# First layer's tokens in three parts of 384 instead of four of 288, with the pairs of heads taken alternately from the two halves of the tokens

## The chip, the cores and the metric

The kernel runs on one core of one Trainium2 chip. What counts is the device time of one execution in microseconds. The kernel before took 1,122.79 us, the median of 3 runs from 1,122.03 to 1,123.74.

The engines have short names: PE (TensorE, the matmuls), ACT (ScalarE), DVE (VectorE), POOL (GpSimd) and SP (SyncE, which issues most DMAs). PE reads its operands from SBUF and writes to PSUM, whose banks hold 512 float32 columns.

## What is computed

Three stages run in one kernel. Attention comes first, over 2 batches x 8 heads x 576 tokens x 64, causal, and mixed with a memory term by a gate per head. Its output is laid out as 1,152 tokens x 512 for a dense layer with a softplus between two matrices (the first layer below). Then come 8 experts, each weighted per token by a matrix P.

```
a = softmax(scale * q @ k.T, causal);  local = a @ v
mem_out = (phi(q) @ M_prev) / (phi(q) . z_prev + 1e-6);  g = 1 / (1 + exp(-beta))    # beta: one number per head
x = g * mem_out + (1 - g) * local                # [2, 8, 576, 64] -> [1152, 512]

h = x @ moe_w_in                                 # [1152, 2048]
y = (max(h, 0) + log1p(exp(-|h|))) @ moe_w_out   # [1152, 512]

P = exp(y @ w_gate - max), 8 times scaled by rows and columns
out = sum over e of P[:, e] * (max(y @ w1[e], 0) @ w2[e])
```

## The kernel before, in words

**Precision.** Every large product is made of three: each float32 operand is split into a rounded high part and the rest (`..h` and `..l`), and `products` issues high x high, high x low and low x high. ACT writes the high part (`copy`, L715), DVE or POOL the low part (`less`, L1029; POOL L655 for part of the experts' weights).

**Attention.** `pairs` runs over 8 pairs of heads (one pair fills 128 partitions), with a schedule written out by hand for each engine. The result of pair p is kept transposed in `xh[:, p, :]` and `xl[:, p, :]`, 576 tokens each. Before, pairs 0 to 3 are batch 0 and pairs 4 to 7 batch 1. ACT starts with three DMAs: two that bring `beta` to all partitions (L706), one per batch, and one for z (L707). Its first op is `gate_t` (L792), which waits for beta; DVE makes `gate_all` and `keep_all` from it (L1124 to L1131) before it takes up its first part of Q, `ql` (L1036). All later ACT ops are queued behind `gate_t`.

**First layer.** The loop is: 2 halves g of the 2,048 hidden features; in each, C1 = 4 chunks c of N1 = 288 tokens; in each chunk 8 tiles s of 128 features. `hidden1` makes the tile h of 128 features x 288 tokens in a bank of `ps_h` (12 matmuls), ACT and DVE compute the softplus (`soft_exp_ln`, `soft_sum`) and split it into `hh`, `hl` (`soft_hi`, `soft_lo`, a ring of 4), and `output1` adds its product with `moe_w_out` to four banks of `ps_y` (12 matmuls). PE's order is `hidden1` of tile n + 2, then `output1` of tile n; that is a step. At the end of a chunk DVE drains the four banks into `acc` (`drain_y`), and the first `output1` of the next chunk waits for that.

**What runs beside it.** The experts' part needs the first 512 tokens of y split in 7 forms (`xah`, `xal`: three quarters as they are, four sums that POOL makes in `token_sums`) and the first weights split (`weights_hi`, `weights_lo`, on POOL `weight_sums` and `weight_sums_lo`). Before, the tokens are split in steps 1 to 7 of the last chunk but one of g = 1 (kind "tokens"), and the weights in steps 1 to 3 of the last (kind "last"). In the last chunk's steps 6 and 7 there are no more tiles to make, and PE does the first products of the experts there: P1, P6, P5 before output 6, P2 and P7 before output 7, then P3 and P4 (`hidden2`). P1 and P2, and P4 with weights w = 2, wait for `c1_lo` of DVE, the others (P6 first) for `c1_los`, which POOL gives after L655. That op waits for part 2 of `weights_hi` on ACT.

The lines where a weight split waits or is waited for:

```
act.wait_ge(c1_sum, 4 * fp + 4)                            # weights_hi, part 2 (L856)
copy(w1c_h[i][:, 3:7, :, :], ws[:, :, :, :]).then_inc(c1_hi, 1)
pool.wait_ge(c1_hi, 3 * fp + 3)                            # weight_sums_lo (L654), then .then_inc(c1_los, 1)
pe.wait_ge(c1_los, 2 * s + i + 1)                          # hidden2, w >= 3 (L1607)
```

Of the kernel before, what the change touches and what calls it, by code (L numbers as in the profile page):

```python
# [12 lines left out]

P = 128
LAG = 2
RING = 4
MASKED = -1.0e30


# [48 lines left out]
def build(nc, q, k, v, M_prev, z_prev, beta, moe_w_in, moe_w_out, moe2_w_gate, moe2_w1, moe2_w2, out):  # L68
    B, H, S, D = q.shape
    DM = H * D  # L70
    KT = DM // P
    T = B * S
# [8 lines left out]
    FT = 8  # L81
    FS = FT * P
    G1 = moe_w_in.shape[1] // FS
    C1 = 4
    N1 = T // C1
    NTT = T // P
    M1 = C1 * FT
# [2 lines left out]
    SK_AT = [(1, "P4"), (2, "P7"), (2, "P4"), (3, "P4"), (4, "P7"), (4, "P4"), (5, "P4"), (6, "P7")]  # L90
    assert len(SK_AT) == SK
    SCALE = D ** -0.5
    assert D == 64 and 2 * D == P and TAIL == 64 and NQ == 9 and N1 * 2 == S and moe2_w1.shape[2] == FS
    NS, NB8, G = 5, 8, 2

    KEYS = [P, 2 * P, 3 * P, 4 * P, S]
# [14 lines left out]
    with ExitStack() as top:  # L111
# [75 lines left out]


        h_work, o = at_("h_work", X1, [P, 4, N1])
        assert 4 * N1 <= 2 * NJ * P  # L190
        W20 = o
        w2h, o = at_("w2h", W20, [P, FT, DM], F32R)
        w2l, o = at_("w2l", o, [P, FT, DM], F32R)
# [77 lines left out]
        BANK = {"P1": bank_a, "P2": bank_a, "P6": bank_b, "P7": bank_b, "P4": bank_b, "P5": bank_c, "P3": bank_c}  # L271
        width = lambda u: NA if u < 2 else NB
        XORDER = [0, 1, 2, 3, 4, 6, 5]
        XDONE = {x: n + 1 for n, x in enumerate(XORDER)}

        QUARTER = {"11": 0, "22": 1, "12": 2, "21": 3}
# [144 lines left out]

        PART_DONE = [1, 1, 2, 2, 3, 4, 5, 6, 8]

        def steps_of(t):

            return slice(2 * t, min(2 * t + 2, 9))
# [2 lines left out]
        @block.sync  # L429
        def _(sp):  # L430
            def load_heads(dst, src, pair, done):
                both = src[bass.ds(2 * pair, 2), :, :]
                for h in range(2):
                    sp.dma_start(dst[:, 0:NT, h * D:(h + 1) * D],
                                 src[bass.ds(2 * pair + h, 1), 0:NT * P, :].rearrange("o (j p) d -> p (o j) d", p=P))                        .then_inc(done, 16)
                sp.dma_start(dst[0:TAIL, NT, :].rearrange("p (h d) -> p h d", h=2),
                             both[:, NT * P:S, :].rearrange("h p d -> p h d")).then_inc(done, 16)

            def load_pair(pair, first=False):

                if first:
                    load_heads(q_nat, q3, pair, ld_q)
                else:
                    sp.wait_ge(phi_z, pair)
                    sp.dma_start(z_nat[:, pair % 2, :], z3[:, pair * P:(pair + 1) * P].broadcast_to([P, P]))\
                        .then_inc(ld_z[pair % 2], 16)
                    sp.wait_ge(t_ready, 5 * pair + 3)
                load_heads(k_nat, k3, pair, ld_k)
                if not first:
                    sp.wait_ge(phi_exp, pair + 1)  # L450
                    sp.wait_ge(phi_relu, pair + 1)
                    load_heads(q_nat, q3, pair, ld_q)
                    sp.wait_ge(v_split, 4 * pair + 4)
                else:
                    sp.wait_ge(nat_zeroed, 1)
                load_heads(v_nat, v3, pair, ld_v)
                for h in range(2):
                    sp.dma_start(mem_nat[h * D:(h + 1) * D, h * D:(h + 1) * D],
                                 m3[bass.ds(2 * pair + h, 1), :, :].rearrange("o p d -> p (o d)")).then_inc(ld_m, 16)
                if pair:  # L460
                    sp.wait_ge(ld_w1, 16 * pair)
                cols = slice(pair * P, (pair + 1) * P)
                sp.dma_start(raw1[:, :, cols], w1_dram(moe_w_in[:, cols])).then_inc(ld_w1, 16)
                sp.dma_start(raw2[:, pair, :], moe_w_out[cols, :]).then_inc(ld_w2, 16)
# [238 lines left out]
        def _(act):  # L703
            b2 = beta.rearrange("(o n) -> o n", o=1)
            for b in range(B):
                act.dma_start(beta_all[:, b * H:(b + 1) * H], b2.broadcast_to([P, H])).then_inc(ld_beta, 16)  # L706
            act.dma_start(z_nat[:, 0, :], z3[:, 0:P].broadcast_to([P, P])).then_inc(ld_z[0], 16)  # L707
            act.preload_act_table_set("natural_log_exp_and_others")
            act.sem_inc(t_hi, 5)
# [181 lines left out]
            def chunk(g, c, kind="", first=False):  # L891
                for s in range(FT):
                    n = g * M1 + c * FT + s
                    head = (s + LAG) % FT
                    ends = kind == "last" and g == G1 - 1
                    if not (ends and s + 1 >= FT):
                        soft_hi(n + 1, s + 1)
                    if not (ends and s + LAG >= FT):
                        soft_exp_ln(n + LAG, s + LAG)
                    if first and head == s + LAG:  # L900
                        split_w2(0, head)
                    if kind == "last" and not ends:
                        for tile in range(0 if s == 0 else s + LAG, min(s + LAG + 1, FT)):
                            split_w1(g + 1, tile, n - s + tile + 1)
                        if s >= 1:
                            split_w2(g + 1, s - 1, n + RING)
                    if kind == "tokens" and s >= 1:
                        if s == 1:
                            act.wait_ge(y_drained, KT * (C1 + 2) + KT)
                        tokens_hi(XORDER[s - 1], 0, NA, xah, xas, xa_sum, xa_hi)  # L910
                    if ends and 1 <= s <= 3:
                        weights_hi(0, 0, s - 1)
                    if ends and s == 4:
                        weights2_hi(0, 0)

            chunk(0, 0, "", True)
# [1 line left out]
                chunk(0, c)  # L918
            chunk(0, C1 - 1, "last")
            split_w2(1, FT - 1, M1 + RING)  # L920
            with act.Fori(0, C1 - 2) as c:
                chunk(1, c)
            chunk(1, C1 - 2, "tokens")
            chunk(1, C1 - 1, "last")

            def scale_first(s, u, tiles):
# [31 lines left out]
            tokens_b(3)  # L958
            copy_logits(2)
            tokens_b(4)  # L960
            copy_logits(3)
            tokens_b(6)
            tokens_b(5)

# [47 lines left out]
        def _(dve):  # L1012
# [232 lines left out]
            def chunk(g, c, kind="", first=False):  # L1245
                for s in range(FT):
# [8 lines left out]
                    if kind == "last" and not ends:  # L1255
                        for tile in range(0 if s == 0 else s + LAG, min(s + LAG + 1, FT)):
                            split_w1(g + 1, tile)
                        if s >= 1:
                            split_w2(g + 1, s - 1)
                    if kind == "tokens" and s >= 1:  # L1260
                        tokens_lo(XORDER[s - 1], 0, NA, xah, xal, xas, xa_sum, xa_hi, xa_lo)
                    if ends and 1 <= s <= 2:
                        weights_lo(0, 0, s - 1)
                    if ends and s == 4:
                        weights2_lo(0, 0)
                if not ends:
                    drain_y(g, c)
# [3 lines left out]
                chunk(0, c)  # L1271
            chunk(0, C1 - 1, "last")
            split_w2(1, FT - 1)
            with dve.Fori(0, C1 - 2) as c:
                chunk(1, c)
            chunk(1, C1 - 2, "tokens")
            chunk(1, C1 - 1, "last")

            sum_u2(0, 0)
# [143 lines left out]
        def _(pe):  # L1423
# [127 lines left out]
            def hidden1(n, slot, c, tile, stage):  # L1551

                pe.wait_ge(h_read, n + 1)
                pe.wait_ge(w1_lo, FT * stage + tile + 1)
                for kt in range(KT):
                    at_ = bass.ds((c // 2) * (HPB * S) + kt * S + (c % 2) * N1, N1)
                    last = products(ps_h[:, slot % 2, 0:N1], (w1h[:, tile, kt, :], w1l[:, tile, kt, :]),
                                    [x[:, :, :].rearrange("p a b -> p (a b)")[:, at_] for x in (xh, xl)],
                                    kt == 0, kt == KT - 1)
                last.then_inc(h_ready, 1)  # L1560
# [205 lines left out]
```

## Time and profile before

| | |
|---|---|
| median of 3 runs | 1,122.79 us |
| profiled execution | 1,121.92 us |
| its span, first to last instruction | 1,120.1 us |
| mean granted clock of PE | 0.998 |
| PE busy | 1,106.3 us, 99% |
| DVE, ACT, POOL busy | 707.2, 502.2, 433.7 us |
| chain that ended last | PE 95%, DVE 2%, issue 1%, POOL 1% |

The span is 1.8 us shorter than the execution's own time; what lies around it isn't in the trace. The share of busy time says which engine is full, and the chain of waits says what each piece of work came after. Along the program there are four stretches: a start up to about 26 us, attention to 146 us, the first layer to 354 us, and the experts. One chunk of the first layer lasts about 25.4 us. A DMA row of the page gives the time from issue to landing, not the time that its packets take.

### The profile page before, as it was taken

To read this page: it belongs to the slowest core of one execution; us is meant where nothing else is said; L and a number is where in the kernel's file an instruction comes from. 1 tells how busy PE (TensorE), PEld (TensorE's weight loads), DVE (VectorE), ACT (ScalarE), POOL (GpSimd) and SP (SyncE) were. 2 spreads that over 40 slices of the span, in tenths; PEclk is the share of its full clock that TensorE was granted. 3 is DMA by queue.
4 is the path that set the end of the run, shared out by engine and by line. 5 is a ranking of instruction groups with operands and counts; after the bars stand their busy time and mean duration, and the time that the engine had idled before them with its cause. 6 is when DMAs were issued, how large, how long until landed. Compare 5 with 4: busy or idle time off the path is not lost.

```text
span 1120.1 us, 21542 instructions
## 1 busy us (share of the span) xinstructions
PE 1106.3 (99%) x7114; PEld 1006.7 (90%) x7114; DVE 707.2 (63%) x1359; ACT 502.2 (45%) x1126; POOL 433.7 (39%) x487
## 2 busy tenths in 40 slices
PE   6999999999999999999999999999999999999998
PEld 4888899999998988999998989989899899898997
DVE  6988743363357787666656667565675656657564
ACT  5888765585566333532333323333233333333331
POOL 6988700000116243353434434244252442524421
PEclk9999999999999999999999999999999999999999
DMA  4343112002001011101111011110111101111001
GB/s 110 92 103 100 38 70 75 1 1 77 0 0 57 20 57 39 57 20 57 57 37 56 19 56 56 37 56 19 56 56 37 50 25 56 50 38 43 19 10 76
DMA packets 65934, 52.79 MB, mean 47 GB/s; under 512 B 32480, under 2 KB 53984, under 8 KB 65888
## 3 DMA queue, kind: packets, MB, share of 16 engines
q1 hardware_dynamic: 65456, 52.13, 15.2%
q8 instruction: 25, 0.41, 0.2%
q14 instruction: 21, 0.17, 0.0%
q10 hardware_dynamic: 432, 0.07, 0.0%
HBM read 49.83 MB, written 2.36 MB: 47 GB/s over the span
## 4 chain that ended last, share of the span: by engine, by line
PE 95%; DVE 2%; issue 1%; POOL 1%; DMA 0%; ACT 0%; SPq 0%; ACTq 0%; POOLq 0%; DVEq 0%
PE ps_y L1464 40%; PE ps_h L1464 27%; PE ps_g L1464 17%; PE ps_o L1464 5%; PE ps_p L1502 2%; PE ps_s L1478 2%; PE ps_y L1696 1%; PE ps_s L1464 0%; DMA k_nat<-in_k_dram 0%; DVE zl L1226 0%; PE ps_t L1445 0%; DVE acc L1345 0%; PE ps_t L1456 0%; PE ps_t L1449 0%; POOL prob L594 0%
## 5 line engine op out<-in xcount | busy, mean ns | idle before, releaser
L889 ACT ACTIVATE zh<-h 128x256 fp32r<-128x256 f32 (+1 forms) x256 | 112.2, 444 | 328.7 <-POOL h L667 133.6
L1464 PE MATMUL ps_y<-w2c_h,zh 128*128 128x512 f32 x512 | 202.7, 396 | 0.0
L1464 PE MATMUL ps_y<-w2c_l,zh 128*128 128x512 f32 x512 | 201.8, 394 | 0.0
L1464 PE MATMUL ps_y<-w2c_h,zl 128*128 128x512 f32 x512 | 199.4, 389 | 0.0
L662 POOL TENSOR_TENSOR h<-u,p 128x256 f32<-128x256 f32 (+1 forms) x64 | 56.9, 889 | 350.6 <-DVE u L1203 350.6
L1226 DVE SCALAR_TENSOR_TENSOR zl<-h,zh 128x256 fp32r<-128x256 f32 (+1 forms) x256 | 173.0, 681 | 8.5 <-ACT zh L889 6.3
L1464 PEld LDWEIGHTS ps_y<-w2c_h,zl 128*128 128x128 f32 x512 | 96.2, 188 | 21.9
L1464 PEld LDWEIGHTS ps_y<-w2c_h,zh 128*128 128x128 f32 x512 | 96.6, 189 | 13.4
L1464 PEld LDWEIGHTS ps_y<-w2c_l,zh 128*128 128x128 f32 x512 | 96.6, 189 | 11.8
L1353 DVE SCALAR_TENSOR_TENSOR acc<-ps_y,weight,acc 128x512 f32<-128x512 f32 x112 | 82.1, 741 | 37.2 <-PE ps_y L1464 37.2
L667 POOL TENSOR_TENSOR h<-h,p 128x256 f32<-128x256 f32 (+1 forms) x64 | 61.0, 952 | 101.3 <-DVE h L1214 101.3
L655 POOL TENSOR_TENSOR w1c_l<-ws,w1c_h 128x1024 fp32r<-128x1024 f32 x32 | 76.8, 2401 | 27.9 <-ACT w1c_h L715 27.9
L1156 DVE SCALAR_TENSOR_TENSOR h_work<-ps_h,h_work 128x288 f32<-128x288 f32 x64 | 29.3, 457 | 88.5 <-ACT h_work L823 88.5
L1464 PE MATMUL ps_h<-xbh,w1c_l 128*128 128x320 f32 x256 | 79.1, 309 | 0.0
L1464 PE MATMUL ps_h<-xbl,w1c_h 128*128 128x320 f32 x256 | 79.0, 309 | 0.0
L1464 PE MATMUL ps_h<-xbh,w1c_h 128*128 128x320 f32 x256 | 78.7, 307 | 0.0
L1464 PE MATMUL ps_h<-xh,w1h 128*128 (+1 forms) x256 | 75.6, 295 | 0.0
L1464 PE MATMUL ps_y<-hh,w2h 128*128 128x288 f32 x256 | 75.5, 295 | 0.0
L1464 PE MATMUL ps_y<-hh,w2l 128*128 128x288 f32 x256 | 75.5, 295 | 0.0
L1464 PE MATMUL ps_h<-xh,w1l 128*128 (+1 forms) x256 | 75.5, 295 | 0.0
L1464 PE MATMUL ps_y<-hl,w2h 128*128 128x288 f32 x256 | 75.4, 294 | 0.0
L1464 PE MATMUL ps_h<-xl,w1h 128*128 (+1 forms) x256 | 75.4, 294 | 0.0
(243 smaller groups left out, 3049.6 us busy)
## 6 DMA issues: line engine op xcount, KB each, us to landing
rc<-in_moe_w_dram SPq DMA_DIRECT2D x64, 512.0 KB, 3.6
out_dram<-acc SPq DMA_DIRECT2D x9, 256.0 KB, 2.0
q_nat<-in_q_dram SPq DMA_DIRECT2D x16, 128.0 KB, 2.5
k_nat<-in_k_dram SPq DMA_DIRECT2D x16, 128.0 KB, 2.9
v_nat<-in_v_dram SPq DMA_DIRECT2D x16, 128.0 KB, 2.4
raw<-in_moe_w_in_dram SPq DMA_DIRECT2D x8, 256.0 KB, 3.0
raw<-in_moe_w_out_dram SPq DMA_DIRECT2D x8, 256.0 KB, 3.1
raw<-in_moe_w_in_dram SPq DMA_DIRECT2D x1, 2048.0 KB, 7.8
```

The costliest lines, as they stand in the source:

```text
L655: pool.tensor_tensor(w1c_l[i][:, 3:7, :, :], ws[:, :, :, :], w1c_h[i][:, 3:7, :, :].bitcast(F32), ALU.subtract).then_inc(c1_los, 1)
L662: pool.tensor_tensor(h22[:, 0:n], u3[:, 0:n], p5[:, 0:n], ALU.add).then_inc(h22_done, 1)
L667: pool.tensor_tensor(h12[:, 0:n], h12[:, 0:n], p5[:, 0:n], ALU.add).then_inc(h12_done, 1)
L889: act.activation(z_place(u, quarter, 0), rows, ACT.Relu).then_inc(e_hi, 1)
L1156: dve.scalar_tensor_tensor(out=h_sp[:, slot % 2, :], in0=ps_h[:, slot % 2, 0:N1], scalar=0.0, in1=h_abs[:, slot % 2, :], op0=ALU.max, op1= ...
L1226: dve.scalar_tensor_tensor(out=z_place(u, quarter, 1), in0=rows[:, 0:n], scalar=0.0, in1=z_place(u, quarter, 0).bitcast(F32), op0=ALU.max, ...
L1353: dve.scalar_tensor_tensor(out=here, in0=y, scalar=weight[:, i, bass.ds(e, 1)], in1=here, op0=ALU.mult, op1=ALU.add).then_inc(z_drained, 1)
L1464: last = pe.matmul(dst, a[x], b[y], start=start and i == 0, stop=stop and i == 2)
L1478: pe.matmul(ps_s[:, bank + h, 0:w], x[r, half, t * P:(t + 1) * P], y[r, half, 0:w], start=i == 0, stop=False)
L1502: last = pe.transpose(ps_p[:, b % 2, at_:at_ + P], rows, ident[:, :])
L1696: last = pe.matmul(bank[0:E, 0:N1], wg[:, kt, :], y1[:, kt, c * N1:(c + 1) * N1], start=kt == 0, stop=kt == KT - 1)
```

## The change

C1 goes from 4 to 3 and N1 from 288 to 384, so the first layer has 48 tiles instead of 64. A chunk of 384 no longer ends where a batch ends (576), so the tokens of both batches must lie one behind the other: pairs are taken as batch 0, batch 1, batch 0, batch 1 (`place_of`), and the pair's number gives its place in `xh`, `xl`. The gates are used by the pair's number, so `beta_all` is filled in that order too: one DMA per batch still, now with a third dimension on both sides. The ring of `hh`, `hl` has 2 places. `h_work` grows from 4,608 to 6,144 bytes per partition. The tokens are split in the last chunk itself, up to two forms in a step (`TOKENS_AT`), and the weights two steps later than before.

```diff
-RING = 4
+RING = 2
-    C1 = 4
+    C1 = 3
-        assert 4 * N1 <= 2 * NJ * P
+        assert 4 * N1 <= 3 * NJ * P
+        TOKENS_AT = [0, 0, 2, 4, 6, 7, 7, 7, 7]
+        def place_of(pair):
+            return pair % B * (NP // B) + pair // B
             def load_heads(dst, src, pair, done):
+                pair = place_of(pair)
...
             for b in range(B):
-                act.dma_start(beta_all[:, b * H:(b + 1) * H], b2.broadcast_to([P, H])).then_inc(ld_beta, 16)
+                act.dma_start(beta_all[:, :].rearrange("p (k b h) -> p k b h", b=B, h=2)[:, :, b, :],
+                              b2.rearrange("o (k h) -> o k h", h=2).broadcast_to([P, HPB, 2])).then_inc(ld_beta, 16)
...
-                    if kind == "tokens" and s >= 1:
-                        if s == 1:
-                            act.wait_ge(y_drained, KT * (C1 + 2) + KT)
-                        tokens_hi(XORDER[s - 1], 0, NA, xah, xas, xa_sum, xa_hi)
-                    if ends and 1 <= s <= 3:
-                        weights_hi(0, 0, s - 1)
-                    if ends and s == 4:
+                    if ends and s == 1:
+                        act.wait_ge(y_drained, KT * (C1 + 2) + KT)
+                    if ends:
+                        for x in XORDER[TOKENS_AT[s]:TOKENS_AT[s + 1]]:
+                            tokens_hi(x, 0, NA, xah, xas, xa_sum, xa_hi)
+                    if ends and 3 <= s <= 5:
+                        weights_hi(0, 0, s - 3)
+                    if ends and s == 6:
                         weights2_hi(0, 0)
...
-                    at_ = bass.ds((c // 2) * (HPB * S) + kt * S + (c % 2) * N1, N1)
+                    at_ = bass.ds(kt * T + c * N1, N1)
```

The same edits stand in DVE's chunk (`tokens_lo`, `weights_lo`, `weights2_lo`); one `copy_logits` goes.

ACT's queue at the end of the first layer, before: from the second part of the first weights to their second matrix (`w1c_h_110<-ws` is part 2 of `weights_hi`; `hh<-h_work` is `soft_hi`, and the three ops on `h_work` are `soft_exp_ln`).

```order
L715 ACTIVATE w1c_h_110<-rc_0_127 128x256
L715 ACTIVATE hh<-h_work 128x288
L819 ACTIVATE h_work<-ps_h 128x288
L821 ACTIVATE h_work<-h_work 128x288
L823 ACTIVATE h_work<-h_work 128x288
L715 ACTIVATE w1c_h_110<-ws 128x1024
L715 ACTIVATE hh<-h_work 128x288
L819 ACTIVATE h_work<-ps_h 128x288
L821 ACTIVATE h_work<-h_work 128x288
L823 ACTIVATE h_work<-h_work 128x288
L715 ACTIVATE w2c_h_132<-rc_0_129 128x1024
L715 ACTIVATE hh<-h_work 128x288
```

The same stretch now:

```order
L723 ACTIVATE w1c_h_110<-rc_0_127 128x256
L723 ACTIVATE hh<-h_work 128x384
L827 ACTIVATE h_work<-ps_h 128x384
L829 ACTIVATE h_work<-h_work 128x384
L831 ACTIVATE h_work<-h_work 128x384
L723 ACTIVATE w1c_h_110<-ws 128x1024
L723 ACTIVATE hh<-h_work 128x384
L723 ACTIVATE w2c_h_132<-rc_0_129 128x1024
L723 ACTIVATE s_119<-ps_h 128x256
L723 ACTIVATE w1c_h_115<-rc_1_128 128x512
L723 ACTIVATE w1c_h_115<-rc_1_128 128x256
L723 ACTIVATE p_120<-ps_h 128x256
```

Before, three `hh` and six ops on `h_work` stood between part 2 and `s_119<-ps_h` (what ACT takes from P1), beside the second matrix; now one `hh` and the second matrix are left between them. Part 2 follows the softplus of the last tile instead of that of the last but two.

ACT's first rows, before:

```order
L706 DMA beta_all<-in_beta_dram 128x8 x2
L707 DMA z_nat<-in_z_prev_dram 128x128
L708 ACT_TABLE_LOAD
L792 ACTIVATE gate_t<-beta_all 128x16
L715 ACTIVATE qh<-ps_t 128x512
```

and now:

```order
L713 DMA beta_all<-in_beta_dram 128x4x2 x2
L715 DMA z_nat<-in_z_prev_dram 128x128
L716 ACT_TABLE_LOAD
L800 ACTIVATE gate_t<-beta_all 128x16
L723 ACTIVATE qh<-ps_t 128x512
```

Nothing moves there; the shape of beta's two loads goes from 128x8 to 128x4x2, and `gate_t` still stands ahead of everything else on ACT.

## Rows read from the trace of the kernel before

**Rows 1.** The page: busy time of PE over the span, its share and matmuls

```profile
PE 1106.3 (99%) x7114; PEld 1006.7 (90%) x7114; DVE 707.2 (63%) x1359; ACT 502.2 (45%) x1126; POOL 433.7 (39%) x487
```

**Rows 2.** Busy time by stage: stretch, us, busy us of each engine, PEclk, DMA

```profile
8.20:11.50 3.30, 3.26 (x12) 2.41 (x12) 1.65 (x4) 2.09 (x7) 0.00 (x0) 0.50 0.62 191
...
26.00:146.25 120.25, 118.91 (x1015) 104.83 (x1014) 100.55 (x239) 97.29 (x274) 98.87 (x153) 1.00 0.37 97
146.25:353.97 207.72, 207.72 (x1567) 207.12 (x1568) 98.57 (x202) 131.94 (x296) 16.66 (x15) 1.00 0.09 29
...
449.30:1117.00 667.70, 667.60 (x3894) 601.83 (x3893) 415.48 (x718) 225.12 (x453) 262.10 (x246) 1.00 0.13 43
```

**Rows 3.** Chain of work in the first layer: start us, us, engine, tile, line, matmuls

```profile
254.89 1.60 PE ps_y L1464 x12
256.49 1.58 PE ps_h L1464 x12
...
328.03 1.78 PE ps_y L1464 x12
```

**Rows 4.** Chain of work later: matmuls of 256, 320 and 512 columns

```profile
345.77 0.72 PE ps_h L1464 x6
346.49 0.72 PE ps_g L1464 x6
...
374.92 0.88 PE ps_g L1464 x6
...
446.55 2.75 PE ps_y L1464 x12
```

**Rows 5.** PE in time, attention stage: pairs of 384 columns, half the rows each

```profile
64.86 0.35 PE L1478 MATMUL ps_s<-kl,qh 64*128 64x384 f32 x2
65.04 0.35 PE L1478 MATMUL ps_s<-kh,ql 64*128 64x384 f32 x2
```

**Rows 6.** ACT in time, last chunk, the step that holds w1c_h<-ws

```profile
337.83 0.41 ACT L819 ACTIVATE h_work<-ps_h 128x288 f32<-128x288 f32 x1 [0.85 <-PE ps_h L1464]
...
339.10 1.04 ACT L715 ACTIVATE w1c_h<-ws 128x1024 fp32r<-128x1024 f32 x1
```

**Rows 7.** POOL in time, from the tokens' sums to the weights' low part

```profile
302.86 1.44 POOL L632 TENSOR_TENSOR xas<-acc 128x512 f32<-128x512 f32 x1 [165.15 <-DVE acc L1243]
...
311.24 1.06 POOL L651 TENSOR_TENSOR ws<-rc,ws 128x256 f32<-128x256 f32 x1
340.22 2.40 POOL L655 TENSOR_TENSOR w1c_l<-ws,w1c_h 128x1024 fp32r<-128x1024 f32 x1 [27.93 <-ACT w1c_h L715]
```

**Rows 8.** All engines in time at the start

```profile
5.29 0.21 ACT L792 ACTIVATE gate_t<-beta_all 128x16 f32<-128x16 f32 x1 [1.84 <-DMA beta_all<-in_beta_dram]
...
6.67 0.18 DVE L1131 TENSOR_SCALAR keep_all<-gate_all 128x16 f32<-128x16 f32 x1
...
8.24 0.69 DVE L1036 SCALAR_TENSOR_TENSOR ql<-ps_t,qh 128x512 fp32r<-128x512 f32 x1 [1.40 <-ACT qh L715]
8.24 1.11 PE L1449 MATMUL ps_o<-ident,k_nat 128*128 128x128 f32 x4 [0.72 <-DMA k_nat<-in_k_dram]
...
10.02 0.69 DVE L1029 TENSOR_TENSOR kl<-ps_o,kh 128x512 fp32r<-128x512 f32 x1 [1.09 <-ACT kh L715]
...
11.42 0.42 PE L1478 MATMUL ps_s<-kh,qh 64*128 64x256 f32 x2
```

**Rows 9.** DMA queues in 1.75 to 5.20 us: packets, MB, share

```profile
q1 hardware_dynamic: 1089, 0.27, 34.9%
q10 hardware_dynamic: 366, 0.05, 7.3%
```

**Rows 10.** DMA issues up to 20 us: count, KB each, median us to landing

```profile
q_nat<-in_q_dram SPq DMA_DIRECT2D x4, 128.0 KB, 2.8
...
z_nat<-in_z_prev_dram SPq DMA_DIRECT2D x1, 64.0 KB, 3.4
beta_all<-in_beta_dram ACTq DMA_DIRECT2D x2, 4.0 KB, 3.4
```

More of the change, by code:

```diff
@@ L92, in build @@
     SCALE = D ** -0.5
-    assert D == 64 and 2 * D == P and TAIL == 64 and NQ == 9 and N1 * 2 == S and moe2_w1.shape[2] == FS
+    assert D == 64 and 2 * D == P and TAIL == 64 and NQ == 9 and N1 * C1 == T and B == 2 and moe2_w1.shape[2] == FS
     NS, NB8, G = 5, 8, 2
@@ L444, in load_pair @@
                     sp.wait_ge(phi_z, pair)
-                    sp.dma_start(z_nat[:, pair % 2, :], z3[:, pair * P:(pair + 1) * P].broadcast_to([P, P]))\
+                    sp.dma_start(z_nat[:, pair % 2, :], z3[:, place_of(pair) * P:(place_of(pair) + 1) * P].broadcast_to([P, P]))\
                         .then_inc(ld_z[pair % 2], 16)
@@ L458, in load_pair @@
                     sp.dma_start(mem_nat[h * D:(h + 1) * D, h * D:(h + 1) * D],
-                                 m3[bass.ds(2 * pair + h, 1), :, :].rearrange("o p d -> p (o d)")).then_inc(ld_m, 16)
+                                 m3[bass.ds(2 * place_of(pair) + h, 1), :, :].rearrange("o p d -> p (o d)")).then_inc(ld_m, 16)
                 if pair:
@@ L920, in _ @@
             split_w2(1, FT - 1, M1 + RING)
-            with act.Fori(0, C1 - 2) as c:
+            with act.Fori(0, C1 - 1) as c:
                 chunk(1, c)
-            chunk(1, C1 - 2, "tokens")
             chunk(1, C1 - 1, "last")
@@ L960, in _ @@
             tokens_b(4)
-            copy_logits(3)
             tokens_b(6)
@@ L1259, in chunk @@
                             split_w2(g + 1, s - 1)
[L1260 to L1264, printed above, removed]
+                    if ends:
+                        for x in XORDER[TOKENS_AT[s]:TOKENS_AT[s + 1]]:
+                            tokens_lo(x, 0, NA, xah, xal, xas, xa_sum, xa_hi, xa_lo)
+                    if ends and 3 <= s <= 4:
+                        weights_lo(0, 0, s - 3)
+                    if ends and s == 6:
                         weights2_lo(0, 0)
@@ L1273, in _ @@
             split_w2(1, FT - 1)
-            with dve.Fori(0, C1 - 2) as c:
+            with dve.Fori(0, C1 - 1) as c:
                 chunk(1, c)
-            chunk(1, C1 - 2, "tokens")
             chunk(1, C1 - 1, "last")
```

## Prediction

> **What bounds the kernel now.** I read the page first: PE is busy 99% of the span [rows 1]. Busy time by stage then says where that is loose [rows 2]. The attention stage after 26 us leaves PE 1.3 us idle in 120, the first MoE layer (146 to 354 us) leaves nothing at a granted clock of 1.00, and the expert loop from 449 us leaves 0.1 in 668. Only the start is loose: from 8.2 to 11.5 us the clock is 0.50, the 1.2 GHz level, and PE there runs fillers while it waits. So a change pays if it takes PE time out of a dense stage, and costs if it puts a wait into one. A late start costs in full as well, since no dense stage can catch up. The third view, the chain of waits, shows pieces of 12 matmuls with nothing between them in the first layer; two of its pieces are late, by 0.15 and 0.19 us [the second is in rows 3], both where a chunk begins and DVE still drains the last one.
>
> **Part 1: 384 columns for 288.** Every tile of the first layer takes 12 matmuls to make (`ps_h`) and 12 to use (`ps_y`). Before, there are 2 x 4 x 8 = 64 tiles, 1,536 matmuls; now 2 x 3 x 8 = 48, 1,152. The columns streamed are the same, 442,368. A piece of 12 at 288 columns takes 1.58 to 1.60 us [rows 3], 132.5 ns each. At the 2.4 GHz of clock 1.00 the columns are 120 ns of that; 12.5 ns are per matmul. The sum before is 1,536 x 132.5 = 203.5 us.
> No row has a full matmul of 384 columns. From below: the same 12.5 ns on top of 160 gives 172.5 ns, 198.7 us, a gain of 4.8. From above: two matmuls of 384 columns on half the rows each follow one another in 0.18 us [rows 5]; 178 ns gives 205.1 us, a loss of 1.6. The nearest rows are the full ones: 320 columns at 0.88/6 = 146.7 ns and 512 at 2.75/12 = 229.2 ns [rows 4]. 384 lies a third of the way: 174.1 ns, 200.6 us. I take this: **-2.9 us**.
> On what a matmul costs beyond its columns the Trainium skill disagrees: "TensorE: Matmul & The Clock Gate", section "Back-to-back issue gap", puts the gap of isolated matmuls at the columns over 2.4 GHz plus about 2.5 ns. By that, 384 fewer matmuls would be worth 1.0 us; the pieces of [rows 3] show five times that overhead where each matmul has its own weights, and the measurement decides.
> The two late pieces of 0.34 us together should go: a step (two pieces) is 4.2 us instead of 3.2, while DVE's work in it grows by a fixed-cost share only, and the chunk before the last has no token splits any more. **-0.3 us**, bounds 0 and -0.4.
> The smaller ring for `hh`/`hl` (2 for 4) costs nothing: the tile n+1 is split after tile n-1 is used, and between lie three pieces of PE work, 6.3 us, against some 1.1 us for the two splits. The waits on `h_read` already hold ACT to that pace. The gate's logits have the same columns in 3 groups as in 4; their fewer instructions are under 0.1 us. Fewer y drains (24 for 32) are hidden either way. The order of pairs changes addresses only, and the first layer's first chunk needs pairs 0, 2, 4 and 6, all done when `hidden1` starts.
>
> **Part 2: the tail of the first layer.** The token splits (14 ops of 512 elements on ACT and DVE) now share the last chunk with the weight splits, and these move from its steps 1 to 3 to steps 3 to 5. What waits for them: PE's product P6, in step 6, needs `c1_los`, which POOL gives after `w1c_h<-ws` on ACT. Before, POOL was done at 340.22 + 2.40 = 342.62 and P6 started at 346.49 [rows 4, 7]: 3.9 us in hand. Two steps later there is none. From the time that the step's `hidden1` ends: ACT starts 0.04 us later, reaches the weights 1.27 us after that [rows 6], plus 3 x 0.08 for three wider ops (96 elements; 0.41 us at 288), copies 1.04, POOL starts 0.08 later and takes 2.40. Together 5.1 us. PE has until then one output piece, 12 x 174 = 2.1 us, and P1, 0.72 [rows 4]: 2.8 us. So P6 waits **+2.3 us**. Bounds: 0 if the weights came otherwise early (I see no way), 3.2 if ACT runs behind. ACT's fullest step (3) has 4 ops of about 0.5, two tokens and one weight split of 0.6, 3.9 us of 4.2; step 4 and 5 are light, so it catches up. POOL's sums for the tokens and weights take 302.86 to 312.3 [rows 7], 9.4 us, and are needed first in step 2, one sum, and last in step 5, 21 us into the chunk: covered. Behind `c1_los` on POOL stand the sums for the second weights, 4.2 us, needed only after P3 and P4 and under the logits. What DVE does in that time (`hl` of tile 7, the weights' low part) has PE's pieces P6, P5 and output 6 as cover.
>
> **Part 3: the start.** ACT's two beta loads were 128 runs of 8 numbers; to interleave the two batches each is now 128 x 4 runs of 2 numbers. The bytes are the same, 4 KB each [rows 10]; the packets go from 256 of 32 B to 1,024 of 8 B. ACT waits for them before its first op: at 5.29 us [rows 8], and this wait was the DMA's. Then DVE makes the gates until 6.85, and only then `ql`, at 8.24. The path that sets the start is not this one but `k_nat`, which lands at 8.2 [rows 8].
> How late may beta be? If ACT starts at T, gates are made at T + 1.6, `ql` and `kl` take 0.69 each, the two `qtl` and the last `kl` 0.7 together, and the first scores (11.42 now) start at about T + 3.7. So the start slips by T - 7.7, and by nothing below.
> T isn't in the trace. From 1.75 to 5.20 us the ACT queue moved 366 packets, 106 per us, beta's among them, beside 1,089 of SP's [rows 9]. Bounds: by bytes, T stays 5.3 and the slip is 0. By count times the whole time to landing (3.45 us x 4 + 1.75 = 15.6), the slip is 7.9. At the queue's rate, 1,024 packets need 9.7 us, T is 11.8 with 0.3 for the last signal, the slip 4.0. In favour of counting packets: a z load of 128 packets, all from one row of DRAM as beta's are, takes 3.4 us to land, while a q load of 512 packets and twice the bytes takes 2.8 [rows 10]. I take the middle one: **+4.0 us**. It is also the largest term and the least certain. PE's fillers end at 11.4, so its clock may fall again to the 1.2 GHz level before the scores; up to 1 us more, not in the sum.
>
> **Sum.** -2.9 - 0.3 + 2.3 + 4.0 = +3.1 us on the profiled execution's 1,121.92 us (its span is 1,120.1): 1,125.0. The median of the runs, 1,122.79, is 0.9 above that execution; carried over, 1,125.9.
>
> **Rivals.**
> A. Beta lands early enough (T below 7.7). For it: both loads are 8 KB together, and in the same stretch SP's queue moved three times as many packets as ACT's [rows 9], so the DMA engines can do more than ACT's queue asked of them. Against it: the rates of [rows 9]. Then -0.9: 1,121.9, no change; with the 384 columns at their lower bound, 1,120.0, faster.
> The Trainium skill speaks for this one: "DMA: Bandwidth & Descriptors", section "Why small descriptors are slow (HBM only)", charges about 3 cycles of a bus per packet and 32 bytes of descriptor, by which 48 more packets on each of 16 engines would be an estimated fraction of a us, and the start would not move. No row here shows packets of 8 bytes.
> B. Packets decide in full and hold up SP's loads too: slip 7.9, +7.0 in all, 1,129.8. For it: SP's queue ran at 316 packets per us beside beta. Against: it lets the fixed part of the time to landing grow with the count, too.
> C. P6 finds its weights ready, and beta is early: -3.2, 1,119.6. Against it stands the order of ACT's work; it needs two errors.
> D. 384 columns cost 178 ns: +4.5 on the forecast, 1,130.4. Only pairs that share the array show it.
>
> **How the numbers follow.** Forecast 0.45, A 0.30, B 0.15, C 0.05, D 0.05. A difference under 0.2%, 2.2 us, can't be told from none: faster is below 1,120.5, slower above 1,125.0. The forecast's case spreads with T, 1,123.5 to 1,128: slower 0.8, same 0.2. A: same 0.75, faster 0.25. B and D slower, C faster. So faster 0.08 + 0.05 = 0.13; same 0.09 + 0.22 = 0.31; slower 0.36 + 0.15 + 0.05 = 0.56. The range takes in most of A and B: 1,119.8 to 1,130.5; the forecast's own is 1,123.5 to 1,128.
>
> **What would show it.** Pieces of 12 at 384 columns take 2.07 to 2.09 us. ACT's `gate_t` starts at about 11.8 us with its wait put down to beta's DMA, and the first scores at 15.5. PE has one wait in the last chunk, before P6, 2.3 us, released by POOL. The expert loop is unchanged. The forecast is wrong if `gate_t` starts before 7.7 us, or if P6 starts right behind P1.

## The result and the profile after

| | before | after |
|---|---|---|
| median | 1,122.79 us (5 runs, 1,122.03 to 1,123.77) | 1,129.84 us (5 runs, 1,127.79 to 1,131.12) |
| span of the profiled execution | 1,120.1 us | 1,127.7 us |
| ratio, after to before | | 1.0061, 95% interval 1.0050 to 1.0073 |

The changed kernel is slower, by 7.05 us in the medians and 7.6 us in the spans of the two profiled executions. PE does a little less work than before and waits more; this is the page, with PE's busy time and the granted clock in 40 slices, to be read beside [rows 1]:

```profile
PE 1105.4 (98%) x6722; PEld 1005.4 (89%) x6722; DVE 700.6 (62%) x1319; ACT 489.3 (43%) x1061; POOL 434.9 (39%) x487
...
PEclk9999999999999999999999999999999999999999
```

The clock reads 9 in all 40 slices of 28 us; what is shorter has to be looked for in smaller stretches. PE's busy time fell by only 0.9 us, which already says that something ate what the wider tiles gave. By stage (stretch, us, then busy us and instructions of PE, PEld, DVE, ACT and POOL, PEclk, DMA share, GB/s), beside [rows 2]:

```profile
8.20:14.60 6.40, 0.00 (x0) 0.02 (x1) 0.42 (x2) 0.22 (x1) 0.00 (x0) 1.00 0.40 84
...
34.00:154.80 120.80, 119.77 (x1020) 105.85 (x1018) 100.63 (x238) 97.97 (x274) 98.85 (x153) 1.00 0.36 95
154.80:361.61 206.81, 204.53 (x1184) 204.19 (x1184) 91.89 (x162) 119.06 (x232) 17.36 (x15) 0.99 0.09 29
```

From 8.2 to 14.6 us PE now does nothing (the 1.00 of its clock there is no reading, see the end). Attention and the first layer are as dense as before, but for 2.3 us in the second.

The chain of waits (start us, us, engine, tile, matmuls), beside [rows 3, 4]:

```profile
161.25 2.08 PE ps_h L1471 x12
...
349.05 2.36 POOL w1c_l L662
351.45 1.65 PE ps_g L1471 x6
354.38 2.29 PE ps_y L1471 x12
```

A piece of 12 matmuls at 384 columns takes 2.08 us, 173.3 ns each, where 288 took 1.59 us. Then the last chunk's P6 (`ps_g`) comes behind a POOL op, and its six matmuls take 1.65 us instead of 0.72; the next output piece takes 2.29 instead of 2.08. PE's longest waits (engine, line, what it waited for, total us, times, longest):

```profile
PE ps_t L1452 <- DMA q_nat<-in_q_dram: 10.2, 1, 10.2
PE ps_g L1471 <- POOL w1c_l L662: 2.3, 1, 2.3
```

And the start, engines in order of time, beside [rows 8]: SP's issue of v, ACT's `gate_t`, PE's first transposes of q, the first scores:

```profile
6.71 4.97 SPq L441 DMA_DIRECT2D v_nat<-in_v_dram  x2
...
13.78 0.22 ACT L800 ACTIVATE gate_t<-beta_all 128x16 f32<-128x16 f32 x1 [10.05 <-DMA beta_all<-in_beta_dram]
...
14.61 1.09 PE L1452 MATMUL ps_t<-ident,q_nat 128*128 128x128 f32 x4 [10.17 <-DMA q_nat<-in_q_dram]
...
18.94 0.58 PE L1485 MATMUL ps_s<-kh,qh 64*128 64x256 f32 x2
```

`gate_t` is 8.5 us late, q itself lands 7.7 us later than before, and the scores start 7.5 us later. The DMA queues in the first stretch of [rows 9] (packets, MB, share of 16 engines' time), and then from 8.2 to 11.5 us:

```profile
q1 hardware_dynamic: 528, 0.13, 16.6%
q10 hardware_dynamic: 331, 0.00, 4.3%
```

```profile
q10 hardware_dynamic: 348, 0.01, 5.4%
q1 hardware_dynamic: 77, 0.02, 2.4%
```

ACT's queue moves about 96 packets per us in the first stretch and 105 in the second, of 8 bytes, as it moved 106 of mostly 32 bytes before. SP's queue fell from 1,089 packets to 528 in the first stretch, and from 1,039 to 77 in the second, with its share of the engines' time at 2.4%: the queue is not busy, it is held up. SP's own issue of v took 4.97 us for two DMAs, against 1.48 us in the kernel before; that its queue did not drain is the likely reason.

Put together from the profiled executions. The first deep attention piece on `ps_o` moved from 40.69 to 48.72 us: +8.0. 1,152 x 173.3 ns against 1,536 x 132.5 is -3.9, two late drains -0.3. P6 started 2.4 us after P1's last matmul would have let it, and behind it the slow clock cost 1.5 (6 matmuls of P6 and 6 of P5 took 2.73 us, start to start, instead of 1.43, at about 0.21 us each but the first, and the output piece lost 0.25 us). The sum is +7.7 us; the spans differ by 7.6.

### The profile page after: what moved, and what is told of

Read it like the earlier page. It is cut to its first block, busy times and chain, and to the rows that moved or that the text cites. A ratio compares the mean times of both kernels' runs of the same rounds, so it can differ in the third digit from the quotient of the medians.

```text
span 1127.7 us, 20453 instructions
## 1 busy us (share of the span) xinstructions
PE 1105.4 (98%) x6722; PEld 1005.4 (89%) x6722; DVE 700.6 (62%) x1319; ACT 489.3 (43%) x1061; POOL 434.9 (39%) x487
## 4 chain that ended last, share of the span: by engine, by line
PE 93%; DVE 2%; issue 1%; DMA 1%; POOL 1%; ACT 1%; SPq 0%; ACTq 0%; POOLq 0%; DVEq 0%
PE ps_y L1471 39%; PE ps_h L1471 26%; PE ps_g L1471 17%; PE ps_o L1471 4%; PE ps_p L1509 2%; PE ps_s L1485 2%; DMA k_nat<-in_k_dram 1%; PE ps_s L1471 0%; PE ps_y L1703 0%; DVE zl L1233 0%; PE ps_t L1452 0%; PE ps_t L1456 0%; DVE acc L1352 0%; PE ps_g L1703 0%; PE ps_t L1463 0%
## 5 line engine op out<-in xcount | busy, mean ns | idle before, releaser
L1471 PEld LDWEIGHTS ps_y<-w2c_l,zh 128*128 128x128 f32 x512 | 96.6, 189 | 11.8
L1163 DVE SCALAR_TENSOR_TENSOR h_work<-ps_h,h_work 128x384 f32<-128x384 f32 x48 | 26.8, 558 | 99.3 <-ACT h_work L831 99.2
L1471 PE MATMUL ps_h<-xah,w1c_l 128*128 128x256 f32 x256 | 72.7, 284 | 0.0
L1471 PE MATMUL ps_h<-xal,w1c_h 128*128 128x256 f32 x256 | 72.6, 284 | 0.0
L1471 PE MATMUL ps_h<-xah,w1c_h 128*128 128x256 f32 x256 | 72.4, 283 | 0.0
L1227 DVE TENSOR_TENSOR h<-ps_g,u 128x256 f32<-128x256 f32 (+1 forms) x64 | 29.3, 458 | 64.5 <-PE ps_g L1471 64.3
L723 ACT ACTIVATE s<-ps_h 128x256 f32<-128x256 f32 (+1 forms) x64 | 26.3, 410 | 97.0 <-PE ps_h L1471 96.9
```

The source lines that it names most:

```text
L723: copy = lambda o, i, **kw: act.activation(o, i, ACT.Copy, **kw)
L1163: dve.scalar_tensor_tensor(out=h_sp[:, slot % 2, :], in0=ps_h[:, slot % 2, 0:N1], scalar=0.0, in1=h_abs[:, slot % 2, :], op0=ALU.max, op1= ...
L1227: dve.tensor_tensor(h21[:, 0:n], bank_b[:, 0:n], u3[:, 0:n], ALU.add).then_inc(h21_done, 1)
L1471: last = pe.matmul(dst, a[x], b[y], start=start and i == 0, stop=stop and i == 2)
```

## The experiments

Two theories had to be told apart from their rivals. One: beta's packets alone made the start late, not the new order of the pairs. Two: the wait for P6 costs more than its own length, since the clock falls behind it. Four runs took the changed kernel apart, four put beta's loads into the kernel before, three followed what these showed. Each is compared with the kernel before on the same chip (medians 1,122.7 to 1,123.0). The edits are cut to the lines that matter; the semaphore counts at their ends are left out.

### Beta in 32-byte runs again, all else changed

```diff
-                act.dma_start(beta_all[:, :].rearrange("p (k b h) -> p k b h", b=B, h=2)[:, :, b, :],
-                              b2.rearrange("o (k h) -> o k h", h=2).broadcast_to([P, HPB, 2]))
+                act.dma_start(beta_all[:, b * H:(b + 1) * H], b2.broadcast_to([P, H]))
...
-            act.activation(gate_t[:, :], beta_all[:, :], ACT.Exp, scale=-1.0)
+            act.activation(gate_t[:, :].rearrange("p (k b h) -> p k b h", b=B, h=2),
+                           beta_all[:, :].rearrange("p (b k h) -> p k b h", b=B, h=2), ACT.Exp, scale=-1.0)
```

> The changed kernel, but beta comes as before (two loads of 128 runs of 32 bytes, 256 packets) and gate_t's access pattern puts the numbers in the new order. Theory S (beta's 1,024 small packets made the start late): gate_t starts at 5.3 us as before, the first scores at 11.4 instead of 18.9, and the time falls by the 8.0 us that the start slipped, to 1,121.9. Rival (the start is late by the new order of the pairs, whose loads come from other places in DRAM): q, k still land late, 1,129.8. The tail of the first layer stays as it is: P6 waits 2.3 us.

Measured: 1,122.75 us (11 runs), ratio to the kernel before 0.9992 (0.9983 to 1.0001). ACT's `gate_t` and the first scores:

```profile
5.49 0.21 ACT L799 ACTIVATE gate_t<-beta_all 128x16 f32<-128x16 f32 x1 [2.03 <-DMA beta_all<-in_beta_dram]
...
11.39 0.39 PE L1486 MATMUL ps_s<-kh,qh 64*128 64x256 f32 x2
```

The time is 0.9 us above what was expected, but the scores start where they did, with the pairs in the new order. So the start's slip was beta's packets, and the rest of the change together is worth nothing that can be told, as the terms -3.9, -0.3, +2.4 and +1.5 add up to -0.3. (In this profiled execution the first deep `ps_o` piece comes at 41.80 us, 1.1 later than in that of the kernel before, and at 41.28 in that of the run with both edits below. The granted clock goes with it: its mean from 11.5 to 34 us is 0.85 here, 0.92 in the run with both edits (whose records of the clock begin at 13.0 us) and 1.00 in the kernel before. So part of this is likely PE's clock in the loose stretches of the start; no run tells the order of the pairs apart from it.)

### Weights split one step earlier, beta still slow

```diff
-                    if ends and 3 <= s <= 5:
-                        weights_hi(0, 0, s - 3)
-                    if ends and s == 6:
+                    if ends and 2 <= s <= 4:
+                        weights_hi(0, 0, s - 2)
+                    if ends and s == 5:
                         weights2_hi(0, 0)
```

(and the same for `weights_lo` and `weights2_lo` on DVE)

> The changed kernel with the first weights split in steps 2 to 4 of the last chunk instead of 3 to 5 (the second matrix in step 5). Beta stays slow. POOL's low part then ends about 1.9 us before P6 is due. Theory W (the wait for it costs 2.3 us itself and about 1.5 more, since PE's clock drops to the 1.2 GHz level behind the wait and the next 18 matmuls run at it): P6 starts right behind P1 at full clock and the time falls by 3.9 us, to 1,125.9. Rival (only the wait counts, the slow matmuls come from something else in that place, such as POOL and DVE at the same memory): it falls by 2.3, to 1,127.5, with P6 still at 0.21 us per matmul of 256 columns.

Measured: 1,125.88 us (10 runs), ratio 1.0024 (1.0014 to 1.0033), 4.0 us below the changed kernel. P1 and P6 in the chain (`ps_h`, `ps_g`, six matmuls each):

```profile
348.55 0.71 PE ps_h L1471 x6
349.26 0.72 PE ps_g L1471 x6
```

P6 starts right behind P1 and both run at 0.12 us per matmul. Four us is the wait and its slow matmuls, not the wait's 2.4 alone. POOL (`ws<-rc`) and DVE (`hl`, `w2c_l`) have the same kind of work beside P6 as in the changed kernel, so the slow matmuls were not theirs.

### Both edits

> Both edits on the changed kernel: beta in 32-byte runs, the weights split one step earlier. What is left of the change against the kernel before is the 384 columns and the later chunk's ends: 1,152 matmuls at 173.3 ns are 199.7 us against 203.5, and two late drains of 0.34 go: 4.1 us below the kernel before, 1,118.7. If the gain of the wider tiles is lost elsewhere too (rival), it stays within 2 us of 1,122.8.

Measured: 1,118.63 us (5 runs), ratio 0.9961 (0.9947 to 0.9974): 4.4 us below the kernel before in the medians. P1 and P6 in the chain:

```profile
341.04 0.71 PE ps_h L1472 x6
341.75 0.72 PE ps_g L1472 x6
```

This is the change without its two costs, and the gain is what 384 fewer matmuls and two drains were reckoned at. Between this run and the first of the four stands only the place of the weight splits: 1,122.75 against 1,118.63, 4.1 us.

### Filler matmuls in the wait

The first experiment's kernel, and between P1 and P6:

```diff
-                        hidden2(0, 0, ("P1", "P6", "P5"))
+                        hidden2(0, 0, ("P1",))
+                        for _ in range(10):
+                            pe.matmul(bank_b[:, :].rearrange("p (k n) -> p k n", k=2), w1c_h[0][:, 0, 0, :],
+                                      xah[:, 0, :, :], start=True, stop=True)
+                        hidden2(0, 0, ("P6", "P5"))
```

> As the first of these four (beta in 32-byte runs, weights late), with ten matmuls of 512 columns between P1 and P6 that write to P6's bank and are thrown away: 2.2 us of PE work, where PE waited 2.3 us. Their results aren't used, so the output is the same. Theory W (the clock drops because PE is idle): P6 starts at the same time as without them but at full clock, and the time is 1.5 us below that kernel. Rival (the matmuls behind the wait are slow for another reason): P6 at 0.21 us per matmul as before, the same time.

Measured: 1,121.46 us (11 runs), ratio 0.9984 (0.9975 to 0.9993); 1.3 us below the kernel without fillers. The fillers' row (ten matmuls of 512 columns, merged), a matmul of P6 behind them, and one of the output piece:

```profile
341.64 2.45 PE L1690 MATMUL ps_g<-xah,w1c_h 128*128 128x512 f32 x10
...
344.37 0.28 PE L1472 MATMUL ps_g<-xal,w1c_h 128*128 128x256 f32 x1
...
345.86 0.34 PE L1472 MATMUL ps_y<-hl,w2h 128*128 128x384 f32 x1
```

The same stretch without fillers: the first matmul of P6, one of P5, one of the output piece and one after it:

```profile
344.55 0.39 PE L1472 MATMUL ps_g<-xah,w1c_h 128*128 128x256 f32 x1 [2.28 <-POOL w1c_l L662]
...
345.65 0.42 PE L1472 MATMUL ps_h<-xah,w1c_l 128*128 128x256 f32 x1
...
347.79 0.52 PE L1472 MATMUL ps_y<-hl,w2h 128*128 128x384 f32 x1
...
349.19 0.33 PE L1472 MATMUL ps_y<-hh,w2h 128*128 128x384 f32 x1
```

With fillers a matmul of 256 columns takes 0.28 us and one of 384 takes 0.34 (start to end; they overlap); without, 0.42 and 0.52, from about 1 us after P6's start until one of 384 is back at 0.33, at 349.19. The granted clock goes with it: 0.50 from 345.5 to 346.8 us without fillers, and 1.00 from 341.6 to 349.4 with them. The 10 useless matmuls save 1.3 us, so it is PE's idling before them, not what other engines do, that makes them slow.

### The kernel before with 8-byte runs of beta

```diff
-                act.dma_start(beta_all[:, b * H:(b + 1) * H], b2.broadcast_to([P, H]))
+                act.dma_start(beta_all[:, :].rearrange("p (k b h) -> p k b h", b=B, h=2)[:, :, b, :],
+                              b2.rearrange("o (k h) -> o k h", h=2).broadcast_to([P, HPB, 2]))
```

Beta's loads are those of the changed kernel, and `gate_t` puts the gates back into the old order.

> The kernel before with nothing changed but beta's loads: 1,024 packets of 8 bytes as in the changed kernel, put in order by gate_t's access pattern. Theory S: gate_t at 13.8 us, q landing at 14.6, first scores at 18.9, total 8.0 us over the kernel before, 1,130.8. Rival (the order of the pairs has a part in the late start): less than that.

Measured: 1,130.07 us (4 runs), ratio 1.0063 (1.0046 to 1.0080), 7.2 us over the kernel before.

```profile
13.66 0.22 ACT L793 ACTIVATE gate_t<-beta_all 128x16 f32<-128x16 f32 x1 [9.94 <-DMA beta_all<-in_beta_dram]
```

The first scores start at 18.67 us. Nothing of the change but these two DMAs gives the whole difference of the result.

### Four times the packets at 32 bytes

```diff
-                act.dma_start(beta_all[:, b * H:(b + 1) * H], b2.broadcast_to([P, H]))
+                act.dma_start(beta_rep[:, b, :, :], b2.unsqueeze(1).broadcast_to([P, 4, H]))
```

> The kernel before with beta loaded four times over: 1,024 packets of 32 bytes, each of the same 32 bytes of DRAM, and gate_t reads the first copy. If the count decides: gate_t at 13.8 us as with 8 bytes, 1,130.8. If it is the small size (8 bytes, below some unit): gate_t no later than by the bytes, 5.3 to 7 us, and no slip.

Measured: 1,130.01 us (2 runs), ratio 1.0064 (1.0044 to 1.0084).

```profile
13.78 0.22 ACT L793 ACTIVATE gate_t<-beta_rep 128x16 f32<-128x16 f32 x1 [10.05 <-DMA beta_rep<-in_beta_dram]
```

The first scores start at 18.66 us. 1,024 packets of 32 bytes are as late as 1,024 of 8, to 0.1 us. Between 8 and 32 bytes the size plays no part; the count does.

### 1,024 more packets: from 128 rows, and from one

Ahead of the beta loads of the kernel before, in the same queue, two DMAs of 128 x 4 runs of 8 bytes; `gate_t` waits for them too. They differ only in the source.

```diff
+                act.dma_start(beta_rep[:, b, :, 0:2], q3[bass.ds(b, 1), 0:P, 0:16]
+                              .rearrange("o p (a c) -> p (o a) c", c=4)[:, :, 0:2])       # 128 rows
+                act.dma_start(beta_rep[:, b, :, 0:2], b2.rearrange("o (k h) -> o k h", h=2)
+                              .broadcast_to([P, 4, 2]))                                   # one row
```

> The kernel before with 1,024 packets of 8 bytes more, issued by ACT ahead of beta's 256, and read from 128 different rows of q (their contents aren't used; gate_t waits for them as well). If many packets from one row of DRAM are slow for that reason (theory H): these pass several times faster than 105 per us, SP's queue is not held up, gate_t starts at 7 to 8 us, slip under 1 us. If any small packet costs the same (rival): gate_t at about 16 us (1,280 packets), slip 10.

Measured: 1,123.29 us (8 runs), ratio 1.0004 (0.9993 to 1.0014). PE's transposes of q, `gate_t`, the scores, and the two queues from 1.75 to 3.45 us, when the extra packets pass, and then from 3.45 to 5.90 us, when beta's 256 do:

```profile
5.09 1.09 PE L1448 MATMUL ps_t<-ident,q_nat 128*128 128x128 f32 x4 [0.65 <-DMA q_nat<-in_q_dram]
...
6.48 0.21 ACT L795 ACTIVATE gate_t<-beta_all 128x16 f32<-128x16 f32 x1 [1.79 <-DMA beta_all<-in_beta_dram]
...
12.16 0.58 PE L1481 MATMUL ps_s<-kh,qh 64*128 64x256 f32 x2
```

```profile
q1 hardware_dynamic: 1045, 0.26, 67.4%
q10 hardware_dynamic: 1049, 0.01, 34.6%
```

```profile
q1 hardware_dynamic: 481, 0.12, 21.5%
q10 hardware_dynamic: 319, 0.02, 7.5%
```

> The same with the extra 1,024 packets of 8 bytes read from one row, beta's. Both theories: gate_t at about 16 us (1,280 packets at 105 per us and 1.8 us at the start, 14, to 16 if they slow at the end), slip 8 to 10 us. Beside the run with 128 rows it tells whether the source decides.

Measured: 1,131.89 us (2 runs), ratio 1.0081 (1.0061 to 1.0101). `gate_t`, the scores, and the queues in the stretch of [rows 9]:

```profile
16.10 0.22 ACT L795 ACTIVATE gate_t<-beta_all 128x16 f32<-128x16 f32 x1 [11.40 <-DMA beta_all<-in_beta_dram]
...
20.84 0.58 PE L1481 MATMUL ps_s<-kh,qh 64*128 64x256 f32 x2
```

```profile
q1 hardware_dynamic: 528, 0.13, 16.6%
q10 hardware_dynamic: 328, 0.00, 4.3%
```

`gate_t` starts even sooner beside the 128 rows than the 7 to 8 us expected. From 128 rows ACT's queue moves 1,049 packets in 1.70 us, 617 per us, while SP's moves 615 per us beside it, and the kernel is no slower. From one row it moves 95 per us in the stretch of [rows 9], and SP's queue falls to 528 packets there, where it has 1,300 beside the 128 rows. One and the same execution shows the turn: as soon as the extra packets are through and beta's own 256 pass, ACT's queue falls to 130 per us and SP's to 196. SP's first load of q, ahead of that, is there 1.8 us sooner than in the kernel before (5.09 against 6.89 us), and k, behind it, 0.7 us later (8.98 against 8.24).

That is the cause: many packets that read the same few bytes of DRAM pass at about 100 per us, at 8 as at 32 bytes, and what is queued beside them passes no better. It is the source that decides, not the count or size of the packets alone. Two things stay open. Every slow load here is also written as a broadcast, with a step of 0 in its source; no run has that step without the repeated address, or the reverse, so these two aren't told apart. And which part of the way is narrow is not shown.

### What beta's packets cost even before

These three stand on the kernel with both edits (1,118.63 us, 4.4 under the kernel before on its chip). They ran on another chip, where the kernel before took 1,122.69 us; against that they are 5.4, 5.0 and 6.7 us faster.

With one load of 128 runs instead of two, and both batches' gates read from it:

```diff
-            for b in range(B):
-                act.dma_start(beta_all[:, b * H:(b + 1) * H], b2.broadcast_to([P, H]))
+            act.dma_start(beta_all[:, 0:H], b2.broadcast_to([P, H]))
```

> The changed kernel with the weights split one step earlier, and with beta loaded once: 128 packets of 32 bytes, both batches' gates made from the one copy by gate_t's access pattern. Theory S2 (every packet that reads beta's row holds up SP's loads, so the 256 of the kernel before cost something too): k lands about 1 us earlier than 8.3, the first scores start at 10.5 instead of 11.5, total about 1,117.7. If 256 such packets are hidden (rival): as with 256, 1,118.6.

Measured: 1,117.31 us (5 runs), ratio 0.9952 (0.9939 to 0.9966). `gate_t`, the transposes of k, the scores:

```profile
3.49 0.21 ACT L798 ACTIVATE gate_t<-beta_all 128x16 f32<-128x16 f32 x1 [0.51 <-DMA beta_all<-in_beta_dram]
...
7.28 0.66 PE L1456 MATMUL ps_o<-ident,k_nat 128*128 128x128 f32 x4 [0.72 <-DMA k_nat<-in_k_dram]
...
9.95 0.58 PE L1485 MATMUL ps_s<-kh,qh 64*128 64x256 f32 x2
```

With one packet, spread by PE:

```diff
+                act.dma_start(beta_row[0:1, :], b2)
...
+            pe.matmul(ps_s[:, 2, 0:H], ones[0:1, :], beta_row[0:1, :], start=True, stop=True)
```

> The same, but beta comes as one packet to one partition and PE spreads it (one matmul with a row of ones, 8 columns, into a bank that the scores use later), so that no packet but z's 128 reads a row over and over. Theory S2: k lands about 2 us earlier, the first scores at 9.5 to 10, total about 1,117.0. Rival: what sets k's landing is SP's own issues and z's packets; within 0.5 us of the run with 128 packets.

Measured: 1,117.66 us (5 runs), ratio 0.9956 (0.9942 to 0.9969).

```profile
5.42 0.18 ACT L800 ACTIVATE gate_t<-ps_s 128x16 f32<-128x16 f32 x1 [2.41 <-PE ps_s L1446]
...
7.12 0.66 PE L1460 MATMUL ps_o<-ident,k_nat 128*128 128x128 f32 x4 [0.67 <-DMA k_nat<-in_k_dram]
...
9.23 0.39 PE L1489 MATMUL ps_s<-kh,qh 64*128 64x256 f32 x2 [0.33 <-issue]
```

And z's load, 128 packets of one row, issued behind ACT's first part of Q, on top of the edit before:

```diff
-            act.dma_start(z_nat[:, 0, :], z3[:, 0:P].broadcast_to([P, P]))
...
+            prep_hi(0, 0, 0)
+            act.dma_start(z_nat[:, 0, :], z3[:, 0:P].broadcast_to([P, P]))
+            prep_hi(1, 0, 0)
```

> The same as the run with PE spreading beta, and z's 128 packets (all from one row too) are issued by ACT after its first part of Q instead of at the start. They are needed by POOL behind phi. Theory S2: the first q and k loads see no such packet, k lands at 5.5 to 6.5 us, the scores start at about 9, total about 1,116.0, unless z then comes too late for POOL. Rival: as without the move.

Measured: 1,115.95 us (5 runs), ratio 0.9943 (0.9929 to 0.9956).

```profile
6.29 1.06 PE L1460 MATMUL ps_o<-ident,k_nat 128*128 128x128 f32 x4
...
9.42 0.58 PE L1489 MATMUL ps_s<-kh,qh 64*128 64x256 f32 x2
```

PE takes up k 1.0, 1.2 and 2.0 us sooner than at the 8.3 us of the kernel with both edits. In the stretch of [rows 9] SP's queue moves 1,073 packets there and 1,746, 1,974 and 2,214 in the three, so each load of this kind that goes helps the queue. The first and the last step help k; the middle one, from 128 packets of beta to one, brings it 0.16 us and no gain in time, which is what its rival expected (within 0.5 us). In the last, k's transposes follow those of q with no wait for the load.

Of the scores' 1.5, 2.2 and 2.1 us the first is kept up to the first deep `ps_o` piece (41.28 us in the kernel with both edits), and 0.7 and 0.9 are left of the others. The granted clock goes with that too: its mean from 11.5 to 34 us is 0.92 in the kernel with both edits and in the first, and 0.85 in the other two. So what the middle one wins at the scores, PE probably loses again at the lower level in a stretch where it often waits. By 0.35 us, between runs that overlap, it wasn't the faster of the first two as expected. The last is the fastest kernel of this study, 6.7 us under the kernel before.

## Why the prediction was right, and where it was off

**The sign and the range held**, at 1,129.84 us in 1,119.8 to 1,130.5; the point, 1,125.9, was 3.9 us low, and the result lies outside the forecast's own 1,123.5 to 1,128. Rival B described the start better than the case that was called likeliest, and the range held because it had been drawn to take in B, at a chance of 0.15. That B's own number, 1,129.8, is met to 0.1 us is partly luck: it has the wider tiles' gain too small by 1.0 us and the slow clock behind P6 at nothing where it cost 1.5, and the two nearly cancel.

**384 columns.** Right in kind. 174.1 ns was taken and 173.3 measured, -3.9 us instead of -2.9. The upper bound from half-array pairs (178 ns) was too high; the constant on top of the columns is 13.3 ns, near the 12.5 of 288. The run with both edits is 4.4 us faster with 384 matmuls fewer. The Trainium skill's 2.5 ns per isolated matmul ("TensorE: Matmul & The Clock Gate", section "Back-to-back issue gap") would have made it 1.0, plus the drains' 0.3: for pieces whose matmuls each bring their own weights the runs do not bear it out.

**P6.** The wait came out as added up, 2.3 us by the view of waits. What wasn't priced is the clock behind it, +1.5 us. In the windows of the changed kernel, PE had 0.17 us of work from 349.0 to 351.4, and the granted clock is 0.50 from 351.4 to 353.1, the 1.2 GHz level:

```profile
349.00:351.40 2.40, 0.17 (x2) 0.00 (x0) 1.99 (x1) 2.40 (x5) 2.35 (x1) 0.98 0.00 0
351.40:353.10 1.70, 1.65 (x7) 1.66 (x8) 1.70 (x2) 0.02 (x1) 1.56 (x2) 0.50 0.00 0
...
356.00:358.00 2.00, 2.00 (x17) 2.00 (x17) 0.42 (x1) 0.12 (x1) 0.10 (x1) 1.00 0.62 178
```

```profile
351.45 0.58 PE L1471 MATMUL ps_g<-xah,w1c_h 128*128 128x256 f32 x1 [2.28 <-POOL w1c_l L662]
...
352.04 0.42 PE L1471 MATMUL ps_g<-xah,w1c_l 128*128 128x256 f32 x1
```

The term "P6 waits +2.3 us" was thus short by 1.5, and the remark that the "clock may fall again" was made for the start alone. The tail as a whole cost 4.1 us (1,122.75 against 1,118.63) and ate nearly all of the gain of the wider tiles.

**The start.** This is the term that was mis-sized: +4.0 against a measured 8.0. The rate of ACT's queue was read rightly (106 per us before, 96 to 105 after) and so was the count; `gate_t` was put at 11.8 and came at 13.78, 2.0 us of the 4.0: the queue carries 1,200 packets, z's 128 and 48 signals among them, and z's pass between beta's last. Another 1.5 us is in "the first scores start at about T + 3.7", and with it in "the start slips by T - 7.7": they started 5.2 us after `gate_t`. The rule takes SP's loads as landing when they did. They don't, q lands after beta (14.6 us), since the packets of one row hold up both queues; and PE, idle for 10 us, does its transposes at 1.09 us for four instead of 0.63. The last 0.5 us came between the scores and the deep pieces. Rival B named the hold-up and got 0.15, as its own reason (the whole time to landing grows with the count) looked weak. A sign of it was in the trace: SP's queue ran at 316 packets per us beside beta [rows 9], and at 820 per us from 5.20 to 8.20 us, when beta was in.

**The ring of 2, the pairs' order, the fewer drains and logits' groups** cost nothing that can be told, as said: a kernel that keeps all of them and only mends the other two is 4.4 us faster than the kernel before.

**Rival A** fell with its rule: 768 more packets of 8 bytes from one row cost 7.2 us, and 1,024 from 128 rows 0.4 us (1,123.29 against 1,122.90), within the noise. The rule that the prediction cites for it (the Trainium skill, "DMA: Bandwidth & Descriptors", section "Why small descriptors are slow (HBM only)") fits the second case, and its reasoning does not reach the first.

## What to carry to other kernels

Count the packets of a load that is broadcast from DRAM, not its bytes: a rearranged destination can multiply them, and at the 100 or so per us of these runs they also hold up the loads beside them. Bring such a row with as few packets as will do (here one load instead of two was enough), or issue it when nothing is awaited.

When a split or a load is moved later, put a price on the first consumer behind it in another engine's queue. Here PE's wait of 2.4 us made the matmuls behind it slow as well, 1.5 us on top.

## What the runs showed of the hardware that was not expected

- Packets that read one small piece of DRAM pass at 95 to 106 per us over all engines, at 8 and at 32 bytes alike; 8-byte packets from 128 rows passed at about 617 per us beside other loads (all read through a broadcast pattern in the slow case, none in the fast one).
- SP's issues take longer with it: two DMAs of v took 4.97 us to issue in the changed kernel and 1.48 in the kernel before.
- After about 2.4 us of idling in a stage that was dense for 200 us, PE ran for 3 to 3.5 us at the lower level, at once in one execution and 0.9 us after the restart in another. Ten matmuls whose results are thrown away prevented it.
- After 10 us of idling, four transposes at 14.6 us took 1.09 us (0.63 at full speed). The changed kernel's window for that time reads a clock of 1.00, but its profile holds no record of the clock before 20.2 us, so that 1.00 is not a reading. The run with 32-byte packets, whose records begin at 4.6 us, has the same 1.09 us and reads 0.50:

```profile
14.60:16.60 2.00, 1.92 (x8) 1.55 (x9) 0.69 (x5) 0.60 (x1) 0.00 (x0) 0.50 0.56 100
```
